# Third round of outputs moved behind the last products of w2, with two reductions in front of it split or shortened

## The reference

```python
x = (g @ w_out), with g = h * sigmoid(h), h = x @ w_in      # 512 -> 2048 -> 512
logits = x @ phi                                            # 3072 x 32 slots
d = softmax(logits, axis=tokens);   slot_input = d.T @ x    # 32 x 512
for e in range(8):                                          # 4 slots each
    h = np.maximum(slot_input[e] @ w1[e], 0.0)              # 512 -> 1024
    slot_out[e] = h @ w2[e]                                 # 1024 -> 512
c = softmax(logits, axis=slots);    return c @ slot_out     # 3072 x 512
```

## Time and profile before

| | us |
|---|---|
| median of 3 runs (465.12, 465.17, 467.6) | 465.17 |
| the profiled execution | 469.86 |
| its span, first to last instruction | 467.9 |
| TensorE busy | 448.6 (96%) |
| VectorE busy | 276.7 (59%) |
| ScalarE busy | 138.9 (30%) |

### The profile page before, as it was taken

One profiled execution on the slowest core, in us unless ns is written; L12 is line 12 of the kernel. 1 busy time (PEld: TensorE's weight loads), 2 busy tenths in 40 slices (PEclk: granted clock), 3 DMA queues, 4 the chain that ended last, 5 costly groups with the idle time before them and its releaser, 6 DMA issues.

```text
span 467.9 us, 12260 instructions
## 1 busy us (share of the span) xinstructions
PE 448.6 (96%) x5438; PEld 332.6 (71%) x5438; DVE 276.7 (59%) x540; ACT 138.9 (30%) x257; POOL 47.4 (10%) x44
## 2 busy tenths in 40 slices
PE   6799999999999999999999999999999999999990
PEld 5699777777876787767777777787677878543560
DVE  4567558765596566766665785568644557541142
ACT  2475233232331322332332323323222222210031
POOL 2576000000000000000000000000000000010000
PEclk9899999999999999999999999999999999999997
DMA  8996232321142143303321132130160479999997
GB/s 293 411 415 276 101 117 88 104 91 54 59 193 72 37 188 102 103 2 102 104 97 49 59 102 61 46 133 1 30 242 0 182 284 424 395 420 422 420 399 295
DMA packets 14820, 81.59 MB, mean 174 GB/s; under 512 B 1584, under 2 KB 1712, under 8 KB 8880
## 3 DMA queue, kind: packets, MB, share of 16 engines
q1 hardware_dynamic: 14768, 80.81, 45.0%
HBM read 74.51 MB, written 6.29 MB: 173 GB/s over the span
## 4 chain that ended last, share of the span: by engine, by line
PE 92%; DMA 3%; DVE 2%; issue 1%; ACT 0%; DVEq 0%
PE h_ps L310 57%; PE o_ps L294 5%; PE lpu_ps L327 5%; PE sx_ps L269 4%; PE lpu_ps L360 4%; DMA qk_sb<-qk 3%; PE sx_ps L360 2%; PE pt_ps L280 2%; PE sx_ps L699 2%; PE h_ps L1013 2%; PE lpu_ps L699 2%; PE h_ps L734 1%; PE h_ps L951 1%; PE o_ps L993 1%; PE lpu_ps L370 1%; PE pt_ps L1013 1%
## 5 line engine op out<-in xcount | busy, mean ns | idle before, releaser
L310 PE MATMUL h_ps<-x_odd,w_pair 128*128 128x512 f32 x576 | 138.3, 394 | 0.0
L310 PEld LDWEIGHTS h_ps<-x_odd,w_pair 128*128 128x128 f32 x576 | 106.3, 188 | 27.8 <-issue 4.6
L545 DVE SCALAR_TENSOR_TENSOR gT<-gT,h_ps 128x512 f32<-128x512 f32 (+1 forms) x108 | 66.1, 612 | 93.1 <-ACT gT L427 93.0
L427 ACT ACTIVATE gT<-h_ps 128x512 f32<-128x512 f32 (+1 forms) x108 | 58.4, 541 | 178.1 <-PE h_ps L310 177.4
L310 PE MATMUL h_ps<-x_even,w_pair 128*128 128x512 f32 x384 | 92.5, 395 | 0.0
L310 PEld LDWEIGHTS h_ps<-x_even,w_pair 128*128 128x128 f32 x384 | 70.9, 188 | 16.8 <-issue 1.7
L555 DVE STREAM_TRANSPOSE gB<-gT 128x512 f32<-128x512 f32 x80 | 56.7, 709 | 1.8
L310 PE MATMUL h_ps<-x_short,w_pair 128*128 128x256 f32 x384 | 51.6, 288 | 1.0 <-DVE gT L545 0.5
L310 PEld LDWEIGHTS h_ps<-x_short,w_pair 128*128 128x128 f32 x384 | 47.7, 192 | 6.0 <-issue 3.6
L529 POOL TENSOR_TENSOR sc<-sc,row_stats 128x512 f32<-128x512 f32 x23 | 24.0, 1044 | 275.0 <-DVE row_stats L523 275.0
L447 ACT ACTIVATE sc<-sc 128x512 f32<-128x512 f32 x23 | 14.6, 633 | 53.2 <-DVE sc L512 49.1
(11 more groups left out here) (193 smaller groups left out, 383.6 us busy)
## 6 DMA issues: line engine op xcount, KB each, us to landing
unit<-w SPq DMA_DIRECT2D x31, 1024.0 KB, 9.6
qk_sb<-qk SPq DMA_DIRECT2D x24, 640.0 KB, 5.4
v_sb<-v SPq DMA_DIRECT2D x24, 512.0 KB, 3.6
out<-unit SPq DMA_DIRECT2D x6, 1024.0 KB, 7.2
w_stage<-w_in SPq DMA_DIRECT2D x4, 1024.0 KB, 12.0
wot<-w_outT SPq DMA_DIRECT2D x4, 1024.0 KB, 12.7
unit<-w_out SPq DMA_DIRECT2D x4, 1024.0 KB, 5.3
unit_acc<-w SPq DMA_DIRECT2D x1, 1024.0 KB, 8.7
```

The source lines that it names most:

```text
L310: last = nc.tensor.matmul(h_ps[k % 2][:, 0:TOKS[b]], w_pair[:, k // 2, w, kc, k % 2 * 128:k % 2 * 128 + 128], x[:, lo, kc, 0:TOKS[b]], sta ...
L427: nc.scalar.activation(gt_of(b, k), h_ps[k % 2][:, 0:TOKS[b]], ACT.Tanh, scale=0.5).then_inc(tanh_done, 1)
L545: nc.vector.scalar_tensor_tensor(out=gt_of(b, k), in0=gt_of(b, k), scalar=1.0, in1=h_ps[k % 2][:, 0:TOKS[b]], op0=ALU.add, op1=ALU.mult).t ...
```

## The change

Four parts, in the order of the diff:

- **u in halves.** The two groups of fold matmuls write columns 0 to 255 into `pt_ps` and columns 256 to 511 into `h_ps[1]`, as 16 matmuls of 256 columns for 8 of 512. ScalarE copies the left half, VectorE the right, of `uf` and again of `uT`; the transposes and the products wait for the half that they read. VectorE's two copies stand ahead of its softmax work on `logits`. `keep_busy` goes from 3 to 2 at both places.
- **Slot inputs turned by the fold.** The four transposes of `si_part` become four matmuls with `fold[:, 0:SLOTS]` as the moving operand, which turn and add in one step; VectorE's reduction becomes a copy of 128 columns. `keep_busy` goes from 3 to 2.
- **Third round.** Round r = 2 no longer stands behind e = 5 of the right half; it stands behind `slot_outputs(pe, 1)`, in the place of `keep_busy(4)`, and ahead of r = 3. `keep_busy` ahead of `slot_outputs` goes from 3 to 2. On VectorE the copies of r = 2 move behind the copies of `slot_outputs`. Rounds 3 and 5 now use set 1 of the banks and the others set 0, and the waits of `outputs` follow that.
- **First store.** SyncE waits for unit 33 ahead of the first store, not for unit 34.

```diff
+        uf_ps, uT_ps = (pt_ps, h_ps[1]), (s_ps, ex_ps)
...
-            return out_sets[1 if r > ROUNDS and (r - ROUNDS) % 2 else 0]
+            return out_sets[1 if r >= ROUNDS and (r - ROUNDS) % 2 == 0 else 0]
...
-            before = r if r <= ROUNDS else r - 1
-            if before:
-                pe.wait_ge(out_act, 2 * before)
-                pe.wait_ge(out_dve, 2 * before)
+            copied = r if r < ROUNDS else r - 1
+            if r and r != ROUNDS:
+                pe.wait_ge(out_act, 2 * copied)
+                pe.wait_ge(out_dve, 2 * copied)
...
-            sp.wait_ge(unit_in[NU - 2], 16)
+            sp.wait_ge(unit_in[NU - 3], 16)
...
             act.wait_ge(uf_mm, 1)
-            nc.scalar.copy(uf[:], pt_ps[:]).then_inc(uf_cp, 1)
+            nc.scalar.copy(uf[:, 0:256], uf_ps[0][:, 0:256]).then_inc(uf_act, 1)
             act.wait_ge(uT_tr, 1)
-            nc.scalar.copy(uT, s_ps[:]).then_inc(uT_done, 1)
+            nc.scalar.copy(uT[:, 0:256], uT_ps[0][:, 0:256]).then_inc(uT_act, 1)
...
             nc.vector.reciprocal(total[:], esum[:]).then_inc(tail_dve, 1)
+            dve.wait_ge(uf_mm, 1)
+            nc.vector.tensor_copy(uf[:, 256:512], uf_ps[1][:, 0:256]).then_inc(uf_dve, 1)
+            dve.wait_ge(uT_tr, 1)
+            nc.vector.tensor_copy(uT[:, 256:512], uT_ps[1][:, 0:256]).then_inc(uT_dve, 1)
...
             dve.wait_ge(si_tr, 1)
-            nc.vector.tensor_reduce(siT.rearrange("p (k s) -> p k s", k=KC),
-                                    s_ps[:].rearrange("p (k j s) -> p k s j", k=KC, j=4), AX.X, ALU.add).then_inc(siT_done, 1)
+            nc.vector.tensor_copy(siT, s_ps[:, 0:KC * SLOTS]).then_inc(siT_done, 1)
...
                 dve_slot_outputs(dve, h)
-                for r in range(ROUNDS * h, ROUNDS * (h + 1)):
+                for r in range(2) if h == 0 else range(2, 2 * ROUNDS):
...
-            for i in range(4):
-                nc.tensor.matmul(pt_ps[32 * i:32 * i + 32, :], foldd, acc[:, i, :], start=True, stop=False)
+            for half in range(2):
+                for i in range(4):
+                    nc.tensor.matmul(uf_ps[half][32 * i:32 * i + 32, 0:256], foldd, acc[:, i, 256 * half:256 * half + 256],
+                                     start=True, stop=False)
             pe.wait_ge(last_u_act, 2)
             pe.wait_ge(last_u_dve, 2)
-            for i in range(4):
-                last = nc.tensor.matmul(pt_ps[32 * i:32 * i + 32, :], fold[:, 0:SLOTS], last_u[:, i, :], start=False, stop=True)
+            for half in range(2):
+                for i in range(4):
+                    last = nc.tensor.matmul(uf_ps[half][32 * i:32 * i + 32, 0:256], fold[:, 0:SLOTS],
+                                            last_u[:, i, 256 * half:256 * half + 256], start=False, stop=True)
             last.then_inc(uf_mm, 1)
-            keep_busy(3, h_ps[0])
-            pe.wait_ge(uf_cp, 1)
+            keep_busy(2, h_ps[0])
             for g in range(4):
-                last = nc.tensor.transpose(s_ps[:, g * 128:(g + 1) * 128], uf[:, g * 128:(g + 1) * 128], ident[:])
+                pe.wait_ge((uf_act, uf_dve)[g // 2], 1)
+                last = nc.tensor.transpose(uT_ps[g // 2][:, g % 2 * 128:g % 2 * 128 + 128], uf[:, g * 128:(g + 1) * 128], ident[:])
             last.then_inc(uT_tr, 1)
-            keep_busy(3, h_ps[0])
-            pe.wait_ge(uT_done, 1)
+            keep_busy(2, h_ps[0])
             for g in range(NF):
+                pe.wait_ge((uT_act, uT_dve)[g // 2], 1)
...
             for kc in range(KC):
-                last = nc.tensor.transpose(s_ps[:, kc * 128:(kc + 1) * 128], si_part[:, kc * 128:(kc + 1) * 128], ident[:])
+                last = nc.tensor.matmul(s_ps[:, kc * SLOTS:(kc + 1) * SLOTS], si_part[:, kc * 128:(kc + 1) * 128],
+                                        fold[:, 0:SLOTS], start=True, stop=True)
             last.then_inc(si_tr, 1)
-            keep_busy(3, h_ps[0])
+            keep_busy(2, h_ps[0])
...
-                if e % 2 and e // 2 < ROUNDS:
+                if e in (1, 3):
                     outputs(pe, 0, e // 2)
-            keep_busy(3, ex_ps)
+            keep_busy(2, ex_ps)
             slot_outputs(pe, 1)
-            keep_busy(4, ex_ps)
+            outputs(pe, 0, 2)
             for i in range(ROUNDS):
                 outputs(pe, 1, i)
```

More of the change, by code:

```diff
@@ L220, in moe_program @@
         last_u_act, last_u_dve, foldd_done = sem("last_u_act"), sem("last_u_dve"), sem("foldd_done")
-        uf_mm, uf_cp, uT_tr, uT_done, si_mm, si_cp, si_tr, siT_done = (
-            sem(x) for x in ("uf_mm", "uf_cp", "uT_tr", "uT_done", "si_mm", "si_cp", "si_tr", "siT_done"))
+        uf_mm, uf_act, uf_dve, uT_tr, uT_act, uT_dve, si_mm, si_cp, si_tr, siT_done = (
+            sem(x) for x in ("uf_mm", "uf_act", "uf_dve", "uT_tr", "uT_act", "uT_dve", "si_mm", "si_cp", "si_tr", "siT_done"))
         ffn1_mm, relu_act, relu_dve, hid_tr, hT_done, hT_zero, ffn2_mm, so_cp, so_mm, so_done = (
```

## The result

The changed kernel has a median of 467.74 us over 20 executions, the kernel before 465.62 over 20 (the 465.17 of the prediction was the median of its first three). The ratio is 1.0036, with a 95% interval of 1.0023 to 1.0049: 1.1 to 2.3 us slower. Two of the 20 executions of the changed kernel, at 602 and 631 us, ran at a mean granted clock of 0.69 and 0.66; they are in its median, which without them is 467.69, and not in the ratio. The loss is within 0.5%, as forecast; its middle, 1.7 us, lies a little above the +0.7 to +1.4 of the prediction's sum.

What follows compares the result with a forecast made beforehand. DMA was taken to bound the tail: the first store behind a hole and those following. Store 2 at 455.6, plus 5.3 to 6.0, plus three at 2.4, gave +0.7 to +1.4; middle +1.1, median 466.3, range 463.6 to 468.1.

Steps and rivals of the forecast that it cites:

- the prediction's sum: End of the kernel: store 2's issue, its landing time and three more stores give 468.1 to 468.8 against 467.4.
- the w2 end does not move: End of w2: unit 35 lands at 450.8 and sets it; the 1.08 us gained becomes a wait for the DMA.
- the move of the third round opens the hole: Tail: store 2 issued 4.2 us later, at 455.6; the 0.5 us hole becomes 3, with four stores behind it.
- Store 5, forecast at +0.1 us against before: Last store's issue: 459.3 against 459.23, since two-engine copying of 1.3 us a round sets the pace.
- folds hidden, first store small: Ahead of w2's right half: folds near -0.2 us, hidden; stores 0 and 1 at most 0.4 us earlier.
- the latency from idle: Store behind the hole in the tail: takes 5.3 to 6.0 us from issue to landing, as read from the trace.
- store 2 at 455.6 plus 5.3 to 6.0 to landing: Tail: first step of the end time; three more stores at 2.4 follow, giving 468.1 to 468.8.
- store 2 lands in under 5 us: Tail: a listed sign that the prediction is wrong, against its 5.3 to 6.0 us to landing.
- The rival with the short latency: Tail: an idle queue gives 4.7 us or less to landing, so no change, 465.2; chance 0.1.
- The Trainium skill's estimate: Store of 1024 KB: about 2.0 us fixed plus bytes at 436 GB/s, 4.4 us; the sum would be 467.2.
- The clock: Rival: the clock falls in TensorE's new 1.1 us wait ahead of e = 7; in all +2.9, 468.1; chance 0.04.
- the shared engines: Rival: store 0, issued sooner, delays unit 35 by up to 2.4 us; +3.5, 468.7; chance 0.06.

Runs made afterwards that it cites:

- the last run: The changed kernel with the first store waiting for unit 34 again, everything else kept: ratio 1.0025 (0.9998 to 1.0052) to the kernel before.

## Why the prediction was right, and where it was not

**Right: the w2 end does not move.** TensorE waits for the last unit, all the work taken out of w2 becomes a wait (2.64 us for 0.35), and unit 35 sets its end.

**Right: the move of the third round opens the hole.** Store 2 was expected at 455.6 in the profile of before, which is 54.1 behind the fold; it was issued at 54.6, 54.0 and 54.05 in three profiles. The hole was put at 3 us with four stores behind it; it took 2.8 us of DMA time. The round back in w2, at either place, is 2.5 to 2.9 us faster than the changed kernel, so the move is the loss. Store 5, forecast at +0.1 us against before, was issued 58.4 behind the fold for 57.7: 0.7 later, half a microsecond of which is unit 35's own landing in this execution. In the two other changed kernels with all six stores it was issued at 57.9, +0.2.

**Right: folds hidden, first store small.** Both folds alone gave no gain, the first store alone -0.2 in the tail, and none in the changed kernel. (The prediction counts 0.145 us for an instruction of `keep_busy`; its row, six in 0.94, gives 0.157. Nothing hangs on it.)

**Wrong: the latency from idle.** The step "store 2 at 455.6 plus 5.3 to 6.0 to landing" failed. A store on idle engines takes 3.9 us, and "store 2 lands in under 5 us" was one of the prediction's own signs of being wrong. The 6.0 of the earlier trace rows goes with an instruction fetch on one engine. The 5.3 of store 0 was taken with unit 35 still landing; with the same start and no fetch near it (the last run) store 0 took 4.9. The rival with the short latency had that part right, and nothing else: no change, 465.2. The Trainium skill's estimate (DMA: Bandwidth & Descriptors, Anatomy of one DMA) of 4.4 us, fitted to another issuing path, was nearer than the range taken from the rows; the measurement, 3.9, is below it. The rival was wrong in leaving the baseline alone: if the 6.0 is not what an idle queue gives, then the end of before, which was 456.59 + 6.0 + 4.8, was itself inflated. With 3.9 at both places, before ends 55.1 + 3.9 + 2 x 2.45 = 63.9 behind the fold and after 54.6 + 3.9 + 3 x 2.45 = 65.9, or 65.3 with the 54.05 of the two other profiles: +1.4 to +2.0. The runs without a fetch in the way bear both out: store 5 landed 63.9 behind the fold in the kernel before without store 2, and 65.4 to 66.0 in the changed kernels. With the fetch in before, as profiled, the two are equal. The 1.7 us measured is what the sums without a fetch give. That the forecast of +1.1 came near it is luck in part: it had two errors of opposite sign, too long a latency for after (5.65 for 3.9, 1.75 us too much) and one of 6.0 in before that an idle queue does not have (2.1 us too much).

**Open.** How often the fetch meets a store in an execution that is not profiled is not known, so the 1.7 us is not split further. The profiles of the kernel before and of its near relatives have tails of 64.9 to 66.3, the changed kernel's 65.8 to 66.4; the means differ by only 0.25 us where the timings differ by 1.5. Part of the loss is in no profile taken here. Nor can the profiles exclude that some of it lies ahead of the tail, since the start of the fold scatters by 4.5 us; that 1.8 us go when one store is left out of the end speaks against a large share. What makes the version with the round back 1.1 us faster than before is open too: up to 0.4 could be the first store's, the folds gave nothing alone, and in both profiles of such versions the fetch was over ahead of store 3's data. In the third version of the kind, with less filler, it was not, and the ratio was 0.9985. That the extra instructions of the folds shift it there was not tried.

**The clock and the shared engines.** Neither happened. The clock was 1.00 through the wait ahead of e = 7, 1.82 us for the weight loads and 1.34 for the matmuls. Unit 35 landed 49.2 behind the fold with the first store sooner and alone, and at 49.25 in before: store 0 did not delay it.

The version to keep is the one with the third round in w2 and the rest of the change, behind e = 5 or e = 6: 0.9970 and 0.9973 of the kernel before, with intervals that stay below 1. The gain is small beside the noise: the near relative with less filler came to 0.9985, and the kernel before against itself to 1.0012.

## What to carry to other kernels

Where the DMA queue is full to the end of a kernel, move nothing that feeds it behind a wait for its own last load: the work taken from the compute engine becomes a wait, and the store that came late leaves the engines idle with all the later stores behind it. A store may come later at no cost as long as the queue still has work when it is issued: 1.2 us later, with the round behind e = 6, changed nothing here, and 4.2 to 4.7 us later, on engines that had run dry, cost the loss. And before a latency is taken from one row as what an idle queue gives, look at what else ran on those engines beside it, and use the same latency for the kernel before.

## What the runs showed of the hardware

- A store of 1024 KB from SBUF on idle or nearly idle engines landed in 3.9 to 4.1 us in six profiles; its data started 0.75 us behind its issue, and each further store behind it took 2.4 to 2.5 us.
- A fetch of instructions occupied one of the 16 DMA engines for 0.9 to 1.6 us, and in the seven profiles with one beside the store, its landing came 1 to 2 us later, though the mean DMA share of 1.00 did not show it. That the fetch is the cause is argued, not shown.
- Two profiles of the same program differ by 3.2 us in the place of their last block, 2.8 of which arise in the first 21 us: the first block's products began at 21.2 and at 18.3. The later one had waited 2.07 us for a load and then run 3.4 us at a clock of 0.50; the other had neither.
